# Taking the tokens without the last expert first: a feed-forward stage that starts beside the last head of a mixture of experts

## The reference

```python
def _moe_ref(x, w_gate, w_noise, noise, w1, w2):
    noisy_logits = x @ w_gate + np.log1p(np.exp(x @ w_noise)) * noise
    top2 = np.argpartition(-noisy_logits, 2, axis=1)[:, :2]
    ...                                    # top2_w: softmax over the two
    for e in range(E):                     # E = 8, w1[e] 512x1024, w2[e] 1024x512
        for k in range(2):
            mask = top2[:, k] == e
            h = np.maximum(x[mask] @ w1[e], 0.0)
            out[mask] += top2_w[mask, k, None] * (h @ w2[e])

def _moe2_ref(x, w_in, w_out, s, b):       # w_in 512x2048, w_out 2048x512
    r = np.maximum(x @ w_in, 0.0)
    return (s * (r * r) + b) @ w_out
```

## Time and profile before

| what | us |
|---|---|
| three runs, median (lowest, highest) | 756.91 (753.92, 757.74) |
| the profiled execution: its own time | 756.24 |
| its span, first to last instruction | 754.6 |
| PE busy (95% of the span) | 715.5 |
| DVE, ACT, POOL busy | 243.1, 215.8, 299.2 |
| mean granted clock of PE, share of full | 0.973 |

### The profile page before, as it was taken

The page is one execution under the profiler, slowest core; times in us unless marked ns, Lnnn a source line. Parts: engine busy times, 40 slices in busy tenths (PEclk is TensorE's granted clock), DMA queues, the critical chain, the costliest instruction groups (busy, mean ns, idle before and its releaser), DMA issues.

```text
span 754.6 us, 10368 instructions
## 1 busy us (share of the span) xinstructions
PE 715.5 (95%) x4062; PEld 576.9 (76%) x4062; DVE 243.1 (32%) x511; ACT 215.8 (29%) x503; POOL 299.2 (40%) x273
## 2 busy tenths in 40 slices
PE   8788867999999999999999798899999999999998
PEld 3467754888888887888889695788888888888886
DVE  3557676521110111121112010565333343232330
ACT  0768861112120311212121110332223223131221
POOL 0001655288848395774889492900220001000000
PEclk9999877999999999999999899899999999999999
DMA  9976977927949295885969582970221001000001
GB/s 232 260 207 182 292 257 247 391 84 279 313 160 395 86 382 160 299 293 186 389 233 307 188 302 94 317 245 1 56 70 43 0 11 47 28 29 1 0 1 56
DMA packets 54648, 134.34 MB, mean 178 GB/s; under 512 B 7490, under 2 KB 9794, under 8 KB 54602
## 3 DMA queue, kind: packets, MB, share of 16 engines
q0 software_dynamic: 31248, 93.32, 36.8%
q1 hardware_dynamic: 22157, 38.05, 15.6%
q10 hardware_dynamic: 1197, 2.36, 1.3%
...
## 4 chain that ended last, share of the span: by engine, by line
PE 85%; DMA 4%; SPq 4%; issue 2%; ACT 2%; POOL 1%; DVE 1%; POOLq 0%; DVEq 0%
PE ps L318 26%; PE ps L319 26%; PE ps L320 26%; DMA v_all<-in_v_dram 2%; PE ps L1211 2%; SPq L299 1%; PE ps L1159 1%; PE ps L1142 1%; PE ps L1092 1%; SPq L333 1%; POOL x_sorted L446 1%; ACT prob L545 1%; PE ps L1300 1%; PE ps L1124 1%; SPq L294 1%
## 5 line engine op out<-in xcount | busy, mean ns | idle before, releaser
L426 POOL TENSOR_TENSOR w_lo<-w_raw,w_hi 128x1024 fp32r<-128x1024 f32 x64 | 153.0, 2424 | 31.5 <-DVE w_lo L745 16.1
L955 DVE SCALAR_TENSOR_TENSOR h_lo<-ps,h_hi 128x448 fp32r<-128x448 f32 (+1 forms) x64 | 38.4, 599 | 239.8 <-ACT h_hi L595 239.8
L318 PE MATMUL ps<-x_hi,w_hi 128*128 128x448 f32 (+1 forms) x256 | 93.0, 363 | 1.2 <-DVE x_lo L949 1.2
L318 PE MATMUL ps<-w_hi,h_hi 128*128 128x512 f32 x232 | 93.3, 402 | 0.0
L319 PE MATMUL ps<-x_lo,w_hi 128*128 128x448 f32 (+1 forms) x256 | 92.6, 362 | 0.0
L595 ACT ACTIVATE h_hi<-ps 128x448 fp32r<-128x448 f32 (+1 forms) x64 | 33.6, 525 | 206.3 <-PE ps L320 206.3
L320 PE MATMUL ps<-x_hi,w_lo 128*128 128x448 f32 (+1 forms) x256 | 92.3, 361 | 0.0
L320 PE MATMUL ps<-w_hi,h_lo 128*128 128x512 f32 x232 | 91.5, 394 | 0.0
L319 PE MATMUL ps<-w_lo,h_hi 128*128 128x512 f32 x232 | 91.4, 394 | 0.0
L318 PE MATMUL ps<-y_hi,w_hi 128*128 128x512 f32 (+1 forms) x200 | 78.0, 390 | 0.1
L320 PE MATMUL ps<-y_hi,w_lo 128*128 128x512 f32 (+1 forms) x200 | 77.7, 388 | 0.0
...
## 6 DMA issues: line engine op xcount, KB each, us to landing
w_hi<-in_w_pieces_dram POOLq DMA_DIRECT2D x64, 512.0 KB, 12.7
...
```

What stands on the lines that cost most here:

```text
L318: pe.matmul(acc, l_hi, r_hi, start=start, stop=False, skip_group_check=True)
L426: pool.tensor_tensor(piece(w_lo, slot, k), piece(w_raw, slot, k), piece(w_hi, slot, k).bitcast(F32), ALU.subtract).then_inc(pieces_split, 1)
L955: dve.scalar_tensor_tensor(out=h_lo[:, at, i % FT, 0:rows], in0=ps[:, i % FT, 0:rows], scalar=0.0, in1=h_hi[:, at, i % FT, 0:rows].bitcast ...
```

## The change

Tokens are put in a new order: those that do not use the last expert (head 7) first, in their own order, and those that do use it from the end backwards. `order_tokens` works out each token's place; POOL writes for each token a row of 32 bytes (the two rows in `y_sorted`, the token's number, the two gates: `pay`) to that place in a new DRAM table `ordered` (12 indirect DMAs), and SP reads the table back into `ord_i`. The feed-forward stage runs through this table: gathers take their rows from it, mixes their gates, and the output rows are scattered to their tokens by indirect DMAs of POOL (`put_out`) from four `osb` buffers, where SP stored them from one. The first chunk holds only tokens that need heads 0 to 6. Its gathers, mixes and turns run during head 7; the 40 products on zeros are gone. `w_in` is loaded in the order of `IN_ORDER` (the even pieces hold the first eight hidden tiles) by POOL (rounded) and SP (raw) and is split by DVE, four pieces in head 7 and four in the first group of chunk 0. `w_out` is loaded when head 7's products are done. PE reads `steps` ahead of head 4, and waits for head 6's copies only if there is overflow. The rows of `y_sorted` at its end are cleared at the start.

```diff
+O_Y, O_TOK, O_GATE, O_N = 0, 2, 3, 8
+LEAST = 2 * N // (E - 1) // 4 * 4 + 4
+IN_ORDER = (0, 2, 4, 6, 1, 3, 5, 7)
...
+    ordered = nc.dram_tensor("ordered", [N, O_N], I32, kind="Internal").ap()
...
+        osb = nc.alloc_sbuf_tensor_at("osb", [P, TPC, DM], F32, offset=top.at)
...
+        ord_i = top.tensor("ord_i", [P, NT, O_N], I32)
+        ord_f = ord_i[:, :, :].rearrange("p t w -> p (t w)").bitcast(F32)
...
             load_rows(head, 0, HEAD)
             sp.wait_ge(tables_ready, 1)
             clear_head(1)
+            sp.dma_start(y_sorted[2 * N - LEAST:2 * N, :].rearrange("(p j) d -> p j d", j=4),
+                         zrow[0:LEAST // 4, :].unsqueeze(1).broadcast_to([LEAST // 4, 4, DM])).then_inc(y_cleared, 16)
             for p in range(E - 1):
                 load_head(p + 1)
                 if p + 2 < E:
                     clear_head(p + 2)
+                if p == 3:
+                    sp.wait_ge(order_put, 16 * NT)
+                    sp.dma_start(ord_i[:, :, :], ordered.rearrange("(t p) w -> p t w", p=P)).then_inc(order_in, 16)
...
+                if p == 0:
+                    sp.wait_ge(y_cleared, 16)
                 store_head(p)
             sp.wait_ge(tables_ready, 2)
...
+            def load_raw(slot, source, k, landed):
+                dst, rows = piece(w_raw, slot, k), source(0, k)
+                if len(rows.shape) == 3:
+                    dst = dst.rearrange("p (k n) -> p k n", n=DM)
+                sp.dma_start(dst, rows).then_inc(landed, 16)
+
+            sp.wait_ge(over_done, 1)
+            for k in IN_ORDER:
+                load_raw(0, w_in_source, k, raw_first[k])
+            for t in range(2):
+                sp.wait_ge(yg_in[t], 32)
+                sp.wait_ge(yraw_in[t], 32)
             store_head(E - 1)
-
-            for t in range(NT):
-                sp.wait_ge(out_read, t + 1)
-                sp.dma_start(out[t * P:(t + 1) * P, :], osb[:, :]).then_inc(stored, 16)
-            sp.wait_ge(stored, 16 * NT)
+            sp.wait_ge(head.y_done, tiles_before(E))
+            for k in range(PIECES):
+                load_raw(1, w_out_source, k, raw_last[k // 2])
...
+            pool.wait_ge(order_ready, 1)
+            for t in range(NT):
+                pool.indirect_dma_start(out=ordered, out_offset=bass.IndirectOffsetOnAxis(place_i[:, t:t + 1], 0),
+                                        in_=pay[:, t, :], in_offset=None).then_inc(order_put, 16)
...
             pool.wait_ge(over_done, 1)
-            load_weights(E, E, 0, w_in_source)
-            split_weights(E, 0)
+            for k in IN_ORDER:
+                load_hi(0, 0, w_in_source, k)
...
+            pool.wait_ge(order_in, 16)
+            pool.wait_ge(head.xb_turned, turns_before(E))
+            pool.wait_ge(head.y_stored, 16 * tiles_before(E - 1))
             for t in range(TPC):
                 gather(t)
-            load_weights(E + 1, E + 1, 1, w_out_source)
-            for t in range(TPC, NT):
-                pool.wait_ge(mix_ready, t - 1)
-                gather(t)
+            pool.wait_ge(head.y_done, tiles_before(E))
+            for k in range(PIECES):
+                load_hi(0, 1, w_out_source, k, hi_last[k // 2])
+            pool.wait_ge(head.y_stored, 16 * tiles_before(E))
+            for c in range(NCHUNK):
+                if c + 1 < NCHUNK:
+                    for t in range((c + 1) * TPC, (c + 2) * TPC):
+                        pool.wait_ge(mix_ready, t - 1)
+                        gather(t)
+                for t in range(c * TPC, (c + 1) * TPC):
+                    put_out(t)
+            for k in range(TPC):
+                pool.wait_ge(stored[k], 16 * NCHUNK)
...
-            act.wait_ge(head.y_stored, 16 * tiles_before(E - 1))
...
                     act.wait_ge(out_done, t + 1)
-                    if not isinstance(t, int) or t >= 1:
-                        act.wait_ge(stored, t * 16)
-                    act.activation(osb[:, :], ps[:, k, :], ACT.Copy).then_inc(out_read, 1)
+                    if not isinstance(c, int) or c >= 1:
+                        act.wait_ge(stored[k], c * 16)
...
-                y_split(k, k)
+            def last_head():
+                p = E - 1
+                for i in range(KF):
+                    up_split(head, p * KF + i, HEADS[p], i)
+                for k in range(TPC):
+                    y_split(k, k)
+                act.wait_ge(head.y_stored, 16 * tiles_before(p))
+                for t, m in enumerate(row_tiles(HEADS[p])):
+                    y_copy(head, tiles_before(p) + t, t, m)
...
+            def token_numbers():
+                link(dve.tensor_reduce(lane[:, 0:1], cst[:, C_TRI:C_TRI + P], AX.X, ALU.add))
+                link(dve.tensor_scalar(lane[:, 1:2], lane[:, 0:1], -1.0, float(P - 1), ALU.mult, ALU.add))
...
+                dve.tensor_scalar(from_end[:, :], tok[:, :], -1.0, float(N - 1), ALU.mult, ALU.add)
+                dve.tensor_copy(pay[:, :, O_TOK], tok[:, :])
...
+            dve.tensor_tensor(pay[:, :, O_Y:O_Y + 2], moved.rearrange("p (t c) -> p t c", c=2), pos_f[:, :, :], ALU.add)
             dve.wait_ge(ge_ready, 1)
...
+            link(dve.reciprocal(from_gap[:, :], gap[:, :]))
+            dve.tensor_copy(pay[:, :, O_GATE].bitcast(F32), from_gap[:, :])
+            dve.tensor_tensor(pay[:, :, O_GATE + 1].bitcast(F32), gate[:, :], from_gap[:, :], ALU.mult)
...
 
+            def order_tokens():
+                rk, us, tmp = (used[:, i, :] for i in range(3))
+                eight = tbh[:, 0:NT, :]
+                last_e = hot_p[:, E - 1, :]
+                link(dve.tensor_tensor(eight, rank_all[:, :, :], bc(last_e, NT, 1), ALU.mult))
+                link(dve.tensor_reduce(rk, eight, AX.X, ALU.add))
+                link(dve.tensor_tensor(eight, chosen[:, :, :], bc(last_e, NT, 1), ALU.mult))
+                link(dve.tensor_reduce(us, eight, AX.X, ALU.add))
+                link(dve.tensor_scalar(lane[:, 0:1], order[:, E - 1:E], float(CAP), None, ALU.mult))
+                link(dve.tensor_tensor(tmp, tok[:, :], rk, ALU.subtract))
+                link(dve.tensor_tensor(tmp, tmp, lane[:, 0:1].broadcast_to([P, NT]), ALU.add))
+                link(dve.tensor_tensor(us, us, from_end[:, :], ALU.mult))
+                dve.tensor_tensor(place_i[:, :], tmp, us, ALU.add).then_inc(order_ready, 1)
...
+                    if p == 0 and i == 3 * FT:
+                        order_tokens()
...
-            do_head(E - 1)
-            dve.memset(ymix[:, 0, 0:1], 0.0).then_inc(mix_free, 1)
...
-                    g0, g1 = gate[:, 0, t:t + 1], gate[:, 1, t:t + 1]
+                    g0, g1 = (ord_f[:, t * O_N + O_GATE + i:t * O_N + O_GATE + i + 1] for i in range(2))
...
+            def split_ffn(slot, k):
+                if slot == 0:
+                    dve.wait_ge(raw_first[k], 32)
+                    dve.wait_ge(hi_in[k], 16 * (E + 1))
+                else:
+                    dve.wait_ge(raw_last[k // 2], 32)
+                    dve.wait_ge(hi_last[k // 2], 32)
+                dve.tensor_tensor(piece(w_lo, slot, k), piece(w_raw, slot, k), piece(w_hi, slot, k).bitcast(F32), ALU.subtract).then_inc(ffn_split, 1)
...
                         dve.wait_ge(glo_ready, n)
                     dve.scalar_tensor_tensor(out=sqr[:, :], in0=relu[:, i % 2, :], scalar=sbb[:, 0:1], in1=relu[:, i % 2, :],
                                              op0=ALU.mult, op1=ALU.mult).then_inc(sqr_ready, 1)
+                    if isinstance(c, int) and c == 0 and g == 0:
+                        split_ffn(0, IN_ORDER[FG + f])
                     if isinstance(c, int) and c == 0 and 1 <= g <= 2:
-                        split_out((g - 1) * FG + f)
+                        split_ffn(1, (g - 1) * FG + f)
                     dve.wait_ge(ghi_ready, n + 1)
+                    if isinstance(c, int) and c == 0 and g == 1 and f == 0:
+                        dve.wait_ge(head.y_stored, 16 * tiles_before(E))
                     dve.scalar_tensor_tensor(out=g_lo[:, g % 2, f, :], in0=sqr[:, :], scalar=sbb[:, 1:2],
                                              in1=g_hi[:, g % 2, f, :].bitcast(F32), op0=ALU.add, op1=ALU.subtract
...
+            def last_head():
+                p = E - 1
+                for i in range(KF):
+                    if i == 4:
+                        split_ffn(0, IN_ORDER[0])
+                        split_ffn(0, IN_ORDER[1])
+                    if i == 6:
+                        split_ffn(0, IN_ORDER[2])
+                        dve.wait_ge(order_in, 16)
+                        mix_tile(0, 0)
+                        mix_tile(0, 1)
+                    up_split(head, p * KF + i, HEADS[p], i)
+                split_ffn(0, IN_ORDER[3])
...
+            pe.wait_ge(tables_ready, 2)
+            steps = overflow_steps(pe)
             for p in range(LONG // 2 * 2, E - 1):
```

(36 more changed lines are left out.)

79 lines of the change are left out of this document (44 added, 35 removed).

## The result

The changed kernel takes 734.67 us in the median of four runs (733.46 to 737.35); the kernel before, run again on the same chip, 756.06 (753.92 to 757.74, four runs). The ratio is 0.9723, with a 95% interval of 0.9684 to 0.9763: 21 us, or 2.8%, faster.

What follows compares the result with a forecast made beforehand. PE was taken to bound the kernel, with waits only at two seams; 7.7 + 17.6 - 1.3 = 24.0 us off the profiled 756.24 gave 732.2, as a median 732.9, with a range of 730.5 to 740.5.

Steps and rivals of the forecast that it cites:

- Seam 1: Between heads 6 and 7: the 5.34 us hole and 2.33 us of slow clock go; gain 7.7 us.
- Rival A: PE's jump between heads 6 and 7 stays visible: 735 to 740 us, fully 739.9; chance 0.14.
- Seam 2: From head 7's end to the first full feed-forward product: 25.09 us shrink to turns and half products; gain 17.6 us.
- The margin is 0 to 1 us: I take 0 stall: In head 7: gathers and mixes come just in time for the turns, so PE's wait counts as 0.
- rival B: Gathers for head 7's turns land late behind weight pieces: 7 us lost, 739.9, or half, 736.4; chance 0.18.
- The table: Twelve scatters before head 2's loads, and small DVE chains in idle time, are all covered: cost 0.
- order_tokens, nine, in front of 6.23 us of idle: DVE's nine small table instructions are covered by the 6.23 us of idle behind them, at no cost.
- C: The 12 scatters take 2.5 us each and PE stands still 5 us at head 2: 738 us; chance 0.03.
- The end: The last tile leaves by POOL's indirect DMA in place of a plain store: cost 1.3 us, bounds 0 and 1.9.
- Nothing else moves: Sign: besides the seams, only the tail after the last product changes, longer by 1 to 2 us.

Runs made afterwards that it cites:

- again: The changed kernel with no edit, run beside the kernel before on one chip: 735.22 us, ratio 0.971.
- gathers_first: The changed kernel with its eight first gathers ahead of half the feed-forward weight traffic and the fourth split ahead of the mixes: 751.64 us, ratio 0.9771.

## Why the prediction was right, and where it wasn't

**Seam 1** was right in size, 7.5 us of 7.7, and in what it says of the waits: with the read ahead of head 4 and the jump taken without the wait for copies ahead of it, neither shows (0.27 us between products, clock 1.00; no gap over 1 us at this seam in any of the eleven traces with the change). That products already handed over cover the jump remains an argument. How the 4.62 us were divided between read and jump, no run separates. Rival A, by which they stay, is out. The rule of the Trainium skill (Runtime: NRT & Kernel Launch, section Instruction fetch mechanics) that gave it its chance, a stall at a taken branch outside the fetched pages, is not refuted by that: such a stall behind queued products would not be seen here.

**Seam 2** was right up to its last assumption. PE's times came true within 2 us (head 7 forecast for 418.7, started at 416.96; half products 5.7 and 5.75 us). The step that failed is "The margin is 0 to 1 us: I take 0 stall". The gathers were reckoned to land at 441.5 and 444, with head 7 at 418.7: 22.8 and 25.3 us into the head. They are bound to the head's start (the first is issued 6.91 us after it in this trace and 6.94 in again), so they moved with the head when it came 1.7 us early, and their mixes start 25.0 and 27.7 us into it. The first turn is free only up to a mix at some 24. So the term that was mis-sized is the time to the landing, by 2.2 us here and 0.8 in again, whose first mix starts at 23.6 and whose first turn does not wait: the margin was real, but some executions use it up. The waits of the first two turns are 1.13 and 0.60 us. The third turn's 0.62 us came from DVE's order: `h_lo`, a split of 1.2 us, `y_lo` and then the mix. An estimate that summed transfers alone didn't see it. It is rival B in small, and gathers_first bears out that the weights' traffic makes the gathers late; whether the order in the queue or the amount on the way does it, isn't separated.

**The table.** "order_tokens, nine, in front of 6.23 us of idle" took durations from DVE's idle rows and did not look at what POOL does in the same stretch, though the earlier trace rows has it: splits from 153.07 for 18.92 us. Five instructions with two SBUF tiles took 1.8 to 2.3 us each in place of 0.17 to 0.26, and 2.0 us came through to PE. The scatters were right as the sum has them: 1.27 us each, head 2's loads at 185.52, no wait of PE for weights. But in some executions TensorE stands still for 5 to 7 us beside them, a price that no rival had. C expected a wait for `w_lo` at head 2 and none came.

**The end** is the worst mis-sized term: 1.3 us forecast within bounds of 0 to 1.9, and 8.0 measured. The bounds compared landings, and the landing was right (2.7 us against a plain 2.0). The failed step is that the execution ends with the landing. In the kernel before, POOL's last transfer lay some 130 us ahead of the end, so no row showed what it costs to end with one; a bound drawn from rows of another situation should have been wider.

**"Nothing else moves"** failed the other way: 6.5 us in the feed-forward stage and 2.4 in the heads, from 128 bytes of placement. The order of instructions doesn't show it; the list of tiles in the diff does.

**The sum.** The profiled execution took 733.46 where 732.2 was forecast, 1.3 us off. What nobody had reckoned with is larger: 6.5, 2.4 and 1.1 us gained, and 6.7 (the end), 2.4 (the operands) and 2.0 us (the table) lost. The seams, 22.7 us of 25.3, were understood. That the rest cancels was luck: without the shift of 128 bytes the same change would by this reckoning have taken 8.9 us more, some 743.5, above the range, and with an end of the price forecast 6.7 us less, some 728, below it. That the first trace has no hold of TensorE beside the scatters was luck as well.
